# Windowed attention ahead of two MoE layers: spans of 38 keys for 32 queries, softmax inside PSUM, heads in separate row tiles

## What is computed

```python
def _attn_ref(q, k, v):                      # q, k, v: (2, 8, 576, 64)
    ...                                      # factor = 4, Sd = 144
    q_d = q.reshape(B, H, Sd, factor, D).mean(axis=3)      # k_d, v_d alike
    out_up = np.repeat(sm_attn(q_d, k_d, v_d), factor, axis=2)
    mask = np.abs(pos[:, None] - pos[None, :]) < factor    # each query sees 7 keys
    scores = np.where(mask, scale * q @ k.T, -1e9)
    attn = exp(scores - max); attn = attn / (attn.sum() + 1e-9)
    return out_up + attn @ v
```

## Time and profile before

| | us |
|---|---|
| median of three executions | 716.66 |
| the three | 710.19, 716.66, 717.99 |
| profiled execution, first to last instruction (span) | 713.5 |
| TensorE busy | 692.6 (97%) |
| VectorE busy | 242.4 (34%) |
| ScalarE busy | 189.0 (26%) |
| GpSimd busy | 174.0 (24%) |

### The profile page before, as it was taken

The page is one execution under the profiler, slowest core; times in us unless marked ns, Lnnn a source line. Parts: engine busy times, 40 slices in busy tenths (PEclk is TensorE's granted clock), DMA queues, the critical chain, the costliest instruction groups (busy, mean ns, idle before and its releaser), DMA issues.

```text
span 713.5 us, 11146 instructions
## 1 busy us (share of the span) xinstructions
PE 692.6 (97%) x3958; PEld 637.2 (89%) x3958; DVE 242.4 (34%) x376; ACT 189.0 (26%) x399; POOL 174.0 (24%) x121
## 2 busy tenths in 40 slices
PE   6899888999999999999999999999999999999997
PEld 6677678999999999998989898999999999989896
DVE  6979928774222322221212122121212121212211
ACT  4757653432111212343111042111241111111010
POOL 5836636661000003546100055000252000000000
PEclk9969969999999999999999999999999999999999
DMA  9545412430000001333100034000050000001001
GB/s 184 115 99 120 128 49 89 147 122 28 1 1 1 0 0 59 118 112 124 59 0 0 1 107 129 0 0 0 3 165 8 0 0 0 0 0 44 15 29 44
DMA packets 66870, 37.48 MB, mean 53 GB/s; under 512 B 32672, under 2 KB 59552, under 8 KB 66848
## 3 DMA queue, kind: packets, MB, share of 16 engines
q1 hardware_dynamic: 66848, 37.19, 18.5%
HBM read 34.82 MB, written 2.36 MB: 52 GB/s over the span
## 4 chain that ended last, share of the span: by engine, by line
PE 89%; DVE 5%; issue 3%; SPq 2%; ACT 1%; DMA 1%; POOL 0%; DVEq 0%; POOLq 0%; ACTq 0%
PE ps L879 42%; PE ps L946 28%; PE ps L930 14%; PE ps L850 1%; SPq L278 1%; PE ps L789 1%; PE ps L854 1%; PE ps L890 1%; DMA k_raw<-k 1%; SPq L258 1%; PE ps L830 1%; PE ps L777 1%; DVE kz L434 1%; DVE mx L643 1%; DVE rse L665 0%
## 5 line engine op out<-in xcount | busy, mean ns | idle before, releaser
L733 DVE SCALAR_TENSOR_TENSOR g_lo<-ps,g_hi 128x384 fp32r<-128x384 f32 x96 | 53.6, 558 | 270.5 <-ACT g_hi L568 270.5
L568 ACT ACTIVATE g_hi<-ps 128x384 fp32r<-128x384 f32 x96 | 47.2, 491 | 297.4 <-PE ps L879 297.4
L397 POOL TENSOR_TENSOR wa_lo<-w_raw,wa_hi 128x1024 f32 (+1 forms) x24 | 57.4, 2399 | 219.6 <-ACT wa_hi L440 219.6
L879 PE MATMUL ps<-x_hi,wa_hi 128*128 (+1 forms) x288 | 97.7, 339 | 2.4 <-issue 2.4
L879 PE MATMUL ps<-x_hi,wa_lo 128*128 (+1 forms) x288 | 97.5, 339 | 0.0
L879 PE MATMUL ps<-x_lo,wa_hi 128*128 (+1 forms) x288 | 97.3, 338 | 0.0
L879 PE MATMUL ps<-x_hi,wb_hi 128*128 (+1 forms) x288 | 96.9, 336 | 0.0
L879 PE MATMUL ps<-x_lo,wb_hi 128*128 (+1 forms) x288 | 96.9, 336 | 0.0
L879 PE MATMUL ps<-x_hi,wb_lo 128*128 (+1 forms) x288 | 96.8, 336 | 0.0
L397 POOL TENSOR_TENSOR wb_lo<-w_raw,wb_hi 128x1024 f32 x24 | 57.5, 2405 | 106.6 <-ACT wb_hi L440 106.6
L713 DVE CAST g_hi<-g_act 128x384 fp32r<-128x384 f32 x48 | 43.5, 906 | 108.3 <-ACT g_act L563 108.3
(11 more groups left out here) (99 smaller groups left out, 1054.8 us busy)
## 6 DMA issues: line engine op xcount, KB each, us to landing
w_raw<-moe_w SPq DMA_DIRECT2D x64, 256.0 KB, 2.8
w_raw<-moe_w_in SPq DMA_DIRECT2D x16, 256.0 KB, 2.8
w_raw<-moe_w_out SPq DMA_DIRECT2D x16, 256.0 KB, 2.9
q_raw<-q SPq DMA_DIRECT2D x16, 144.0 KB, 3.6
k_raw<-k SPq DMA_DIRECT2D x16, 144.0 KB, 3.7
v_raw<-v SPq DMA_DIRECT2D x8, 288.0 KB
out<-o_acc SPq DMA_DIRECT2D x9, 256.0 KB, 2.0
v_win<-v SPq DMA_DIRECT2D x56, 35.0 KB
```

The costliest lines, as they stand in the source:

```text
L397: pool.tensor_tensor(lo[:, at, :].rearrange("p o n -> p (o n)"), w_raw[:, s, :], hi[:, at, :].rearrange("p o n -> p (o n)").bitcast(F32), ...
L568: act.activation(g_hi[:, f % GB, :], ps[:, HB + f % 4, 0:NB], ACT.Relu).then_inc(relu_done, 1)
L733: dve.scalar_tensor_tensor(out=g_lo[:, f % GB, :], in0=ps[:, HB + f % 4, 0:NB], scalar=0.0, in1=g_hi[:, f % GB, :].bitcast(F32), op0=ALU.m ...
L879: ins = pe.matmul(dst, w[:, f % HALF, c], x[:, kt, at], start=(kt == 0 and i == 0), stop=(kt == KT - 1 and i == 2))
```

## The change

Only the attention is rewritten.

- Windows: 18 spans of 38 keys for 32 queries in place of nine of 70 for 64. Four windows stand above each other in the partitions, so a score tile has 2 heads x 5 x 38 = 380 values in a partition, not 700.
- The scores stay in their two PSUM banks, one for each head: mask, maximum, subtraction, exponential and sum work there in place; the last multiplication writes the probabilities to SBUF. `scores` of the next pair therefore waits for `pl_ready`.
- k is stored once (kT, no zero half, kd likewise). Each head's matmuls take 64 rows of the array: `scores` is 36 matmuls of 38 columns, `scores_down` four of 144, `values` 36 of 32 columns and four of 144, with the heads alternating. `turn_local` makes five of 128 columns, both heads in one.
- Evacuations are merged: q in one copy on ScalarE, k in one on VectorE, the result in one addition. q and k, and the probabilities, now pass through the same two banks one after the other, with a semaphore of its own for each.
- The scaled negative maximum moves from VectorE to ScalarE (L451), the scaling of the down-sampled probabilities from ScalarE to VectorE (L620).
- v windows come with six DMAs for a pair in place of nine, of 48 rows a window and head. All steps are written out; the loop over the middle pairs is gone.

```diff
-        kz = asb("kz", [P, 2, 2, S + 2 * (R - 1)])
+        kT = asb("kT", [P, 2, S + 2 * PAD])
...
-        sm = asb("sm", [P, 2 * GT, W])
-        pl = asb("pl", [P, 2, 2 * GT, W])
+        pl = asb("pl", [P, 2, GT, 2, HS])
...
+                for h in range(2):
+                    src, p0 = v_heads[2 * n + h], HS * h
+                    inner = bass.AP(tensor=src.tensor, offset=src.offset + (GQ - PAD) * D,
+                                    ap=[[D, ROWS], [GQ * D, G - 2], [1, D]])
+                    sp.dma_start(v_win[p0:p0 + ROWS, par, 1:G - 1, :], inner).then_inc(vw_in[par], 16)
+                    sp.dma_start(v_win[p0 + PAD:p0 + ROWS, par, 0, :], src[0:ROWS - PAD, :]).then_inc(vw_in[par], 16)
+                    sp.dma_start(v_win[p0:p0 + S - last, par, G - 1, :], src[last:S, :]).then_inc(vw_in[par], 16)
...
+            def evac_pd(n):
+                par = n % 2
+                act.wait_ge(pd_turned, n + 1)
+                copy(pdT[:, par, 5:8, :], ps[0:HQ, TB, 0:3 * HQ].rearrange("p (c i) -> p c i", i=HQ))\
+                    .then_inc(pd_out, 1)
...
+                sc = local_scores(0, LC)
+                act.activation(sc, sc, ACT.Exp, scale=SCALE).then_inc(exp_done, 1)
...
+                act.activation(nbd[:, :], mxd[:, :], ACT.Copy, scale=-SCALE_D).then_inc(nbd_done, 1)
...
+                dve.tensor_tensor(local_scores(0, LC), local_scores(0, LC), m, ALU.add).then_inc(dve_step, 1)
...
+                dve.tensor_tensor(pl[:, par, :, :, 0:W].rearrange("p t h j -> p h t j"), scores_view(), per_score(rr),
+                                  ALU.mult).then_inc(pl_ready, 1)
...
+                dve.tensor_tensor(pd[:, par, :, :], pd[:, par, :, :],
+                                  rrd[:, :].unsqueeze(2).to_broadcast([HQ, 4, SD]), ALU.mult).then_inc(pd_ready, 1)
...
+            def turn_q(n):
+                pe.wait_ge(q_in[n % 2], 32 * (n // 2 + 1))
+                if n >= 3:
+                    pe.wait_ge(p1_out, n - 2)
+                    pe.wait_ge(pd_out, n - 2)
...
+            def turn_k(n):
+                pe.wait_ge(k_in[n % 2], 32 * (n // 2 + 1))
+                pe.wait_ge(q_out, n + 1)
...
+            def turn_p(n):
+                pe.wait_ge(pl_ready, n + 1)
+                pe.wait_ge(k_out, min(n + 3, N))
...
+                for t in range(GT - 1):
+                    ins = turn_local(n, 0, t * P, t)
+                ins.then_inc(p0_turned, 1)
+                turn_local(n, 1, 0, GT - 1)
+                pe.wait_ge(pd_ready, n + 1)
+                for i in range(5):
+                    ins = turn_down(n, 1, P + i * HQ, i)
+                ins.then_inc(p1_turned, 1)
+                pe.wait_ge(p0_out, n + 1)
+                for i in range(3):
+                    ins = turn_down(n, 0, i * HQ, 5 + i)
+                ins.then_inc(pd_turned, 1)
...
+            def scores(n):
...
+                if n >= 1:
+                    pe.wait_ge(pl_ready, n)
...
+                for g in range(G):
+                    t, c = g // QP, g % QP
+                    for h in range(2):
+                        rows = slice(D * h, D * h + D)
+                        ins = pe.matmul(ps[GQ * c:GQ * c + GQ, SLB + h, t * W:t * W + W],
+                                        qT[rows, par, GQ * g:GQ * g + GQ], kT[rows, par, GQ * g:GQ * g + W],
+                                        start=True, stop=True)
...
+                for turn_over in range(2):
+                    for i in range(G // 2):
+                        for h in range(2):
+                            bank = (turn_over + h) % 2
+                            g = bank * (G // 2) + i
+                            p0, t, c = HS * h, g // QP, g % QP
+                            pe.matmul(ps[D * h:D * h + D, OUTB + bank, i * GQ:i * GQ + GQ],
+                                      v_win[p0:p0 + W, par, g, :], plT[p0:p0 + W, par, t, GQ * c:GQ * c + GQ],
+                                      start=True, stop=True)
```

More of the change, by code:

```diff
@@ L15 @@
 P = 128
-GQ = 64
+GQ = 32
+HS = 64
+ROWS = 48
 RAW = 2
@@ L173, in program, with stage, x_of @@
         block = ctx.enter_context(nc.Block())
[L181 to L205, removed]
-        EARLY = {1: 0, 2: 1, N: 2, N + 2: 3}
[L210 to L229, removed]
+        VW = 6 * 16
+        def stage(n, do):
+            if 0 <= n < N:
+                do(n)
+        EARLY = {1: 0, 2: 1, N: 2, N + 2: 3}
+        def x_of(x, n):
+            return x[:, n % KT, (n // KT) * S:(n // KT) * S + S]
         def tile1(blk, f):
@@ L284, in step @@
+            def step(s):
+                stage(s, load_qk)
+                if s == N:
                     for u in range(RAW, 2 * RAW):
@@ L297, in load_unit @@
                 sp.dma_start(w_raw[:, slot, KT * P:UNIT], second).then_inc(raw_in[slot], 16)
-            steps(sp, step, 2)
+            for s in range(N + 2):
+                step(s)
             with sp.Fori(2, FT1 // RAW) as i:
@@ L340, in _ @@
[L340 to L346, removed]
+            pool.wait_ge(ident_set, 1)
+            pool.wait_ge(edges_zero, 2)
+            for c in range(QP):
+                m = mask[GQ * c:GQ * c + GQ, :, :]
+                if c:
+                    pool.wait_ge(mask_set, c)
+                pool.affine_select(out=m, in_=m, compare_op=ALU.is_ge, fill=NEG, base=0,
+                                   pattern=[[0, GT], [1, W]], channel_multiplier=-1).then_inc(mask_set, 1)
@@ L399, in low_unit, with step @@
                                    ALU.subtract).then_inc(w_ready, 1)
[L401 to L407, removed]
+            def step(s):
+                stage(s, down_qk)
+                stage(s - 2, down_v)
+                stage(s - 4, x_low)
+                if s in EARLY:
+                    u = EARLY[s]
+                    low_unit(u + 1, slice(u, u + 1), areas[0], u % RAW)
+            for s in range(N + 4):
+                step(s)
             def low_units(u0, area, skip=0):
@@ new lines, in x_high, with step @@
+            def x_high(n):
+                act.wait_ge(xf_done, n + 1)
+                copy(x_of(x_hi, n), xf[:, n % 2, :]).then_inc(xhi_done, 1)
+            def step(s):
+                stage(s, evac_q)
+                stage(s - 4, x_high)
+                if s == N:
+                    stage(s - 2, evac_p01)
+                stage(s - 1, exp_local)
+                if s == N:
+                    stage(s - 1, exp_down)
+                if s != N:
+                    stage(s - 2, evac_p01)
+                if s == N + 2:
@@ L574, in end1 @@
                     copy(x_hi[:, j, bass.ds(blk * NB, NB)], ps[:, ACCB + j, 0:NB]).then_inc(x2hi_done, 1)
-            steps(act, step, 4)
+            for s in range(N + 4):
+                step(s)
             AHEAD = len(EARLY)
@@ L716, in hidden1 @@
                                   ALU.subtract).then_inc(g_ready, 1)
-            steps(dve, step, 3)
+            for s in range(N + 3):
+                step(s)
             dve.wait_ge(pr_in, 16)
@@ L819, in scores, with turn @@
-            def scores(duo, par):
-                for bank in range(2):
-                    pe.wait_ge(tp_free[bank], tp_before_qk(duo, par) + 2)
-                if late(duo, par, 1):
-                    pe.wait_ge(masked, 2 * pair(duo, par))
+            def turn(n, raw, bank, last_of):
+                for c in range(3):
+                    ins = pe.transpose(ps[:, TB + bank, c * TP:(c + 1) * TP],
+                                       raw[:, n % 2, 3 * bank + c, :, :].rearrange("p h d -> p (h d)"),
+                                       ident[0:TP, 0:TP])
+                return ins
```

569 lines of the change are left out of this document (257 added, 312 removed).

## The result

| | before | after |
|---|---|---|
| median of four executions, us | 713.42 (708.64 to 717.99) | 734.14 (727.53 to 736.52) |
| profiled execution, span, us | 713.5 | 734.7 |
| mean granted clock of that execution | 0.978 | 0.923 |

The change makes the kernel slower: ratio 1.032, 95% interval 1.027 to 1.037. The forecast was 703 with a range of 691 to 722. What came is the fourth rival, the clock at half (726), and 8 us more. The profiled execution is the slowest of the four (736.52 us by the device's time).

What follows compares the result with a forecast made beforehand. VectorE was taken to bound the middle of the attention. Savings of 15.3 us less 2 for a clock drop left 13.3 off the 713.5 us span, 700.2; adding 3.2 for the median gave 703, range 691 to 722.

Steps and rivals of the forecast that it cites:

- the fourth rival: Middle attention steps: small tiles with pauses keep the clock at half, 14.3 us a step, 726 us; chance 0.09.
- VectorE's step: VectorE's operations in one attention step: 6.7 us, against 10.5 before, at most 8.2.
- The loop: Path through TensorE and ScalarE in a middle attention step, from sharing two banks: 9.4 us a step.
- The tail from the first four turns on: End of an attention step: four turns and wait 0.8 us, then ScalarE's copies and exponentials 3.4 us.
- The loads, put at nothing: DMA loads during attention: a tenth more bytes in a shorter step, costed at nothing.
- the middle choice of 25 ns: Upper part of values, 72 matmuls a pair: 25 ns each, 1.8 us, between bounds of 1.25 and 5.1.
- `scores` at 1.8: TensorE's `scores`, 72 matmuls for 18: 1.8 us at 25 ns each, bounds 0.7 and 5.1.
- half a step of the loop's TensorE part: Allowance for one clock drop in TensorE's short attention pauses: some 2 us, from 4.9 us at full rate.
- 2 off: From `in1` to the last values, 18.7 us: shorter values and turns save 2 us.
- the 8.4 us behind stay: Stretch from the attention's last values to the `out1` at 118.3 us: 8.4 us, taken as unchanged.
- The third: Values and `scores` matmuls keep 70 ns whatever their size, 5.0 us each; 748 us; chance 0.07.
- The second: No tiles side by side, values at 35 ns a matmul, 11.6 us a step; 718 us; chance 0.17.

Runs made afterwards that it cites:

- the first experiment: Changed kernel plus idle transposes ahead of `turn_q`, during the q copy and ahead of the first two `scores`: 706.87 us, ratio 0.996.
- the last run: Changed kernel plus idle transposes in all pauses, the first MoE units' split brought forward and pd's copy earlier on ScalarE: 701.50 us, ratio 0.987.
- the run without b: Changed kernel plus ten idle transposes ahead of `turn_q` and ten ahead of the early `scores`, none during the q copy: 710.81 us, ratio 1.002.

## Why the prediction was wrong

**What held.** VectorE: 548 to 561 ns a tile of 380 (forecast 555), 753 to 759 for the k copy, the maximum below, the final addition and the pd multiplication (750), 166 to 217 for the small ones (220). So pd at the rate of the subtraction was the right end of its bounds. VectorE's step is 25.37 us in four, 6.3 against 6.7. The loop: 9.66 us against 9.4 once the clock is up. Its pieces, forecast and measured there: `turn_q` and wait 0.86, 0.84; q copy 0.64, 0.66 and 0.02; `turn_k` and wait 0.65, 0.83; `scores_down` 0.6, 0.65; values above 1.8, 2.22; below 0.65, 0.64. The tail from the first four turns on was forecast 0.8 + 3.4 = 4.2 and is 3.8. The loads, put at nothing, stand nowhere in the chain of the changed kernel's first 126 us. The upper values were the one piece with a wrong rule: the heads' tiles do run side by side, but halving the moving columns gave nothing, and only the middle choice of 25 ns (31 measured) kept the error at 0.4 us. `scores` at 1.8 was far too dear: 72 matmuls take 1.08 us even at half clock, since eight tiles run side by side.

**What failed.** The step "one of them may drop its clock as now; half a step of the loop's TensorE part ... is some 2", and the 0.09 given to the fourth rival. The sum has 2 us for a clock that in fact stood at half from 14 to 124 us: 23.1 us in the five middle steps alone. I carried the 1.00 of the earlier trace rows over to the changed kernel, where nothing stood for it: the list of matmuls and the pauses between them are new.

The account to 734.7, each against the forecast of 700.2:

- Mask of pair 2 at 26.5 for 24.4: 2.1. The clock was 0.64 from 10 to 26 us already.
- Five steps of 14.27 for 9.4: 24.4. Of these 5 x (14.27 - 9.66) = 23.1 are the clock's, as the first experiment shows, and 1.3 the loop's.
- From that mask to `in1` 10.1 us for 6.5: 3.6, also at 0.50.
- From `in1` to the first `out1` of all, 107.9 to 126.3, 18.4 us; before it is 91.2 to 109.8, 18.6. I had put 2 off: 1.8.
- Behind it 608.4 us for 603.7: 4.7. TensorE waits for late weights once more (3.02 us), and stands at 0.89 for some 15 us after that.
- Less the allowance of 2.

The sum is 700.2 + 36.6 - 2 = 734.8. The fifth line is one that no step of mine and no rival had: "the 8.4 us behind stay" took the `out1` at 118.3 for the first. A first block of `out1` runs at 109.80 in before, and ahead of the second TensorE waits 1.86 us for g_lo. The chain there runs through VectorE, from the last xf over the probabilities to g_lo; ahead of 146.20 in the changed kernel it runs through a load of weights, which lands at 139.6. `in1` and the weights' split stand in fixed places of the lists of ScalarE and GpSimd, so a shift of one against the other opens a wait. The run with the split brought forward shows it closed; no run separates it from the clock in the changed kernel itself.

The fourth rival had the mechanism and the step (14.3 for 14.27). It missed 8 us of the median and 12.0 of the span (its sum adds 3.2 to a span, where here the median lies 0.6 below it). The 12.0 are the slow start (1.9), the slow stretch up to `in1` (3.6), the 2 off behind it (1.8) and the rest with the weights (4.7). It gave small tiles with pauses as the reason. The runs bear out that idle transposes in the pauses raise the clock in most steps, though not in all: it still falls for 3 us in each step of the last run. But 93% busy at 0.50 in the run with ScalarE's new order, and 85% at 1.00, in the run without b (8.31 of 9.75 us, the step from 50.8) and with the values on half their weight columns (29.87 of 35.0 us, 37 to 72), say that TensorE's busy share does not tell the level. What does is open: the transposes differ from the kernel's own work in filling pauses and in using all 128 rows and columns, and no run here parts the two.

**The other rivals.** The third (70 ns a matmul whatever its size) is out: values start 31 ns apart on average, scores 11. The second (no tiles side by side) is out: eight tiles run beside each other in `scores`, and in values the two diagonal ones start 7 ns apart and take together the 58 ns that one matmul took before. That its 35 ns for a matmul of values lies near the 31 measured is chance, since the moving columns do not set them. The Trainium skill's page TensorE: Matmul & The Clock Gate (Wait — 56ns, not 53.3ns?) has a floor of about 25 ns from start to start; this trace does not agree across tiles, with 72 scores in 0.8 us at full clock in the first run. The drain at a change of tiling mode, which the Trainium skill's page TensorEngine Tiling (Key Properties) names, is at most some 0.1 us here: in the run with narrow weights 122 ns pass from the last value above to the first one below, where pairs of the ones above start every 32 ns and pairs of the ones below, in their steady part, every 123.

**What the rewrite is worth.** Each execution lists its mean granted clock. In the run with all idle transposes, executions at 0.981 to 0.984 take 705.2 to 707.6 us; of before, on three chips, those at 0.981 to 0.984 take 709.7 to 715.3. So the rewrite does save some 6 us at an equal clock, where 15.3 were forecast without the clock. The last mask is 7.4 us earlier (78.0 for 85.4) in place of 14: the step from pair 2 to 3 takes 13.4 us (24.33 to 37.69) and not 9.4, the last one 11.4, each with a drop of the clock, the first with the short form of the pause above (0.56), the last with a slow pd as well. That it was slower as it stood is the clock's doing.

## What to carry over

That TensorE runs at full rate in a stage does not carry over to the stage after a rewrite of its matmuls: before splitting them into narrow tiles or putting them behind a copy, price the whole stretch at half clock too, and give that case a chance that fits how little the old rows say of it. A step's chain, read from rows of similar operations, can be forecast to a few tenths of a us; the clock and the work queued behind the changed stage decide what is left of it. Where a stage gets shorter, ask which loads and splits stand at fixed places behind it, and move them with it.

## Not expected of the hardware

- Idle full-size transposes, 15 in a step of TensorE, make a step 4.6 us shorter (9.66 for 14.27). Ten of them, ahead of `turn_q`, brought a clock back that had been at half for 10 us.
- Half clock at 93% busy (the run with `evac_pd` early), full clock at 85% (the run without b).
- `scores`, 64 rows by 32 weight columns: the first eight start within some 50 ns at half clock, 72 take 1.08 us. Values, 38 rows by 64 weight columns: two every 107 ns at half clock and 58 at full, set by the weight columns.
- A pause of 0.3 to 2.4 us at one place of TensorE's list, beside a 16 KB load of instructions, and the clock down behind the long ones.
- GpSimd beside VectorE: an operation on 72x4 values in SBUF takes 1.82 us for 0.17; the multiplication of pd in the first experiment took 1.94 once for 0.76.
